# Routing of tokens to experts: a list built on one engine, four token tiles in one counting product, and a new order of steps

## What is computed

```
logits = x @ w_gate                      # 3072 x 8
order = argsort(-logits.flatten())
for idx in order:                        # best pairs first
    tok, e = idx // E, idx % E
    if assigned[tok] >= 0 or counts[e] >= cap:   # cap = 3072 / 8 = 384
        continue
    assigned[tok] = e; counts[e] += 1
for e in range(E):
    h = maximum(x[mask_e] @ w1[e], 0)    # 384 x 1024
    out[mask_e] = h @ w2[e]
```

## Time and profile before

| | |
|---|---|
| median of three runs | 1098.96 us (1096.31 to 1099.07) |
| the profiled execution's own time | 1096.0 us |
| its span, first to last instruction | 1094.1 us |
| attention and MLP end, routing begins | about 713 us |
| first product of expert 0 | 750.48 us |
| last product of expert 7 | 1090.1 us |
| PE busy, share of the span | 96% |

### The profile page before, as it was taken

The page is one execution under the profiler, slowest core; times in us unless marked ns, Lnnn a source line. Parts: engine busy times, 40 slices in busy tenths (PEclk is TensorE's granted clock), DMA queues, the critical chain, the costliest instruction groups (busy, mean ns, idle before and its releaser), DMA issues. The chain is left out here.

```text
span 1094.1 us, 20341 instructions
## 1 busy us (share of the span) xinstructions
PE 1051.4 (96%) x7545; PEld 899.0 (82%) x7545; DVE 596.2 (54%) x2182; ACT 460.4 (42%) x1172; POOL 422.1 (39%) x472
## 2 busy tenths in 40 slices
PE   8899999999999999999999999948999998999998
PEld 7688888888888888888888888837777786878987
DVE  6754747474746465655656554366665765654110
ACT  5765444444444444444444432303333333334442
POOL 1363222222222222222222224206387547486873
PEclk9999999999999999999999999959999999999999
DMA  6663112121212121212111000014244343323520
GB/s 197 209 205 134 56 56 74 53 71 41 70 55 74 55 68 40 71 55 72 51 63 38 29 11 20 1 29 175 90 161 164 125 164 118 128 104 124 203 107 29
DMA packets 24594, 98.20 MB, mean 90 GB/s; under 512 B 4352, under 2 KB 6400, under 8 KB 22304
## 3 DMA queue, kind: packets, MB, share of 16 engines
q0 software_dynamic: 9824, 58.99, 15.3%
q1 hardware_dynamic: 14672, 37.91, 10.6%
HBM read 84.30 MB, written 12.85 MB: 89 GB/s over the span
## 5 line engine op out<-in xcount | busy, mean ns | idle before, releaser
L427 POOL TENSOR_TENSOR g_low<-g,g_high 128x256 fp32r<-128x256 f32 x192 | 155.1, 808 | 470.8 <-ACT g_high L646 470.7
L536 PE MATMUL up_ps<-x_high,w_high 128*128 128x256 f32 x768 | 227.7, 296 | 0.0
L536 PE MATMUL up_ps<-x_low,w_high 128*128 128x256 f32 x768 | 216.1, 281 | 0.0
L536 PE MATMUL up_ps<-x_high,w_low 128*128 128x256 f32 x768 | 215.1, 280 | 0.0
L814 DVE SCALAR_TENSOR_TENSOR g<-g,up_ps 128x256 f32<-128x256 f32 x192 | 80.4, 419 | 237.0 <-ACT g L639 237.0
L646 ACT ACTIVATE g_high<-g 128x256 fp32r<-128x256 f32 x192 | 80.3, 418 | 209.8 <-PE down_ps L549 140.6
L536 PEld LDWEIGHTS up_ps<-x_high,w_high 128*128 128x128 f32 x768 | 144.5, 188 | 10.7 <-issue 7.7
L549 PE MATMUL down_ps<-w_high,g_high 128*128 128x512 f32 x384 | 152.1, 396 | 0.6 <-POOL g_low L427 0.6
L549 PE MATMUL down_ps<-w_high,g_low 128*128 128x512 f32 x384 | 151.4, 394 | 0.0
L549 PE MATMUL down_ps<-w_low,g_high 128*128 128x512 f32 x384 | 151.2, 394 | 0.0
L536 PEld LDWEIGHTS up_ps<-x_low,w_high 128*128 128x128 f32 x768 | 144.8, 188 | 2.7
(11 more groups left out here) (224 smaller groups left out, 1826.8 us busy)
## 6 DMA issues: line engine op xcount, KB each, us to landing
qk_t<-qk_rows SPq DMA_DIRECT2D x20, 720.0 KB, 4.3
v_w<-v_win SPq DMA_DIRECT2D x40, 232.0 KB
w_raw<-weights SPq DMA_DIRECT2D x16, 512.0 KB, 5.5
x_rest<-x_any POOLq DMA_DIRECT2D x24, 256.0 KB, 3.0
x_rows<-x POOLq DMA_DIRECT2D x12, 512.0 KB, 3.2
w_raw<-gate_rows SPq DMA_DIRECT2D x1, 2048.0 KB, 7.2
qk_t<-qk_rows SPq DMA_DIRECT2D x3, 512.0 KB, 4.5
v_w<-v_win SPq DMA_DIRECT2D x8, 128.0 KB
```

The lines of the kernel that those rows point to most:

```text
L427: pool.tensor_tensor(g_low[:, u % 2, :], g[:, u % 2, :], g_high[:, u % 2, :].bitcast(F32), ALU.subtract)\
L536: last = nc.tensor.matmul(up_ps[:, u % 2, 0:GT * P], a[:, f, w], x[:, grp % 2, c, :], start=k == 0, stop=k == 3 * C - 1)
```

## The change

- **Lists.** `keep_list` writes the list to `token_index` by four reductions, one per 32 partitions, in every round. `tokens_kept`, SP's DMAs, PE's spreading product, the masks in `Tables` and `keep_first_tokens` go.
- **Counts.** From round 1 on four tiles make one product (`PACK` = 128 / 32 = 4): 6 products of 128 x 32 in place of 12 of 64 x 16. The result lies in four diagonal blocks, which `find_reached` joins by three subtractions.
- **Digits per expert.** The maximum over experts moves behind the digit's product: `enough` (in bf16) says for each mark and expert whether it is reached, the product gives 8 digits, and `move_key` takes their maximum (`digit`) first. In the last level `margins` keeps the differences, which `count_wins` multiplies in place of `enough`.
- **Places.** `gaps_of` has new distances; there are two slots from count to digit from round 2 on. The lists stand at 0.37, 1.30, 2.23, 3.16, 4.9, 5.2 and 5.15. From SUMS to LIST there are 7 slots, where there were 9 or 11.
- **GpSimd.** w1 is fetched ahead of f = 5, 4, 2 for experts 1 to 3 and of f = 1 after, tokens ahead of f = 8, 6, 5 and 3.
- `keep_busy(17)` stands behind LIST, where it stood behind NEXT.

```diff
@@ -1254,23 +1235,19 @@
...
-        counts_at = route_ps[0:2 * REACH, 0:2 * E]
-        first_counts = route_ps[0:REACH, 0:E]
-        second_counts = route_ps[REACH:2 * REACH, E:2 * E]
-        digit_at = route_ps[:, 16:17]
-        wins_at = route_ps[:, 32:32 + 2 * E]
+        counts_at = route_ps[:, 0:PACK * E]
+        digit_at = route_ps[:, 32:32 + E]
+        wins_at = route_ps[:, 40:40 + 2 * E]
...
-        spread_at = route_ps[:, 256:256 + COLUMNS]
...
-        second_known = sem("second_known")
-        margin_known = sem("margin_known")
+        digit_found = sem("digit_found")
...
@@ -1312,14 +1286,10 @@
...
         def gaps_of(r):
-            ends = [2, 4] + [4, 1, 1] + [3 if r in (1, 3) else 5, 1, 2]
+            ends = [2, 3] + [3, 1, 1] + [2, 1, 2]
             if r == 1:
-                return [4, 2] + [2, 1] * (UPPER - 1) + [3, 1] + [2, 1] * (NL - UPPER - 1) + ends
-            if r == 2:
-                return [5, 1] + [3, 1] * 2 + [2, 1] * (UPPER - 3) + [3, 1] + [2, 1] * (NL - UPPER - 1) + ends
-            if r == 3:
-                return [5, 1] + [3, 1] * (UPPER - 1) + [4, 1] + [2, 1] * (NL - UPPER - 1) + ends
-            return [5, 2] + [3, 1] * (UPPER - 1) + [4, 1] + [3, 1] * (NL - UPPER - 1) + ends
+                return [2, 2] + [3, 1] * (UPPER - 2) + [2, 1, 3, 1] + [2, 1] * (NL - UPPER - 1) + ends
+            return [4, 2] + [3, 2] * (UPPER - 2) + [2, 2, 3, 2] + [2, 2] * (NL - UPPER - 1) + ends
...
@@ -1375,10 +1345,7 @@
...
-                if p == 0:
-                    pool.wait_ge(token_index_ready, 1)
-                else:
-                    pool.wait_ge(tokens_moved, 16 * BLOCKS * p)
+                pool.wait_ge(token_index_ready, p + 1)
...
@@ -1394,9 +1361,9 @@
...
-                if p + 1 < E and f == {0: FC, 1: 4}.get(p, 0):
+                if p + 1 < E and f == {0: FC, 1: 5, 2: 4, 3: 2}.get(p, 1):
                     fetch_w1(p + 1)
-                if p + 1 < E and f == {0: FC, 1: FC, 2: 6}.get(p, 0):
+                if p + 1 < E and f == {0: FC, 1: FC, 2: 6, 3: 5}.get(p, 3):
                     fetch_tokens(p + 1)
...
@@ -1429,17 +1396,6 @@
...
-        @block.sync
-        def _(sp):
-
-            for r in range(1, E):
-                sp.wait_ge(tokens_ready, r + 1)
-                if r > 1:
-                    sp.wait_ge(tokens_moved, 16 * BLOCKS * (r - 1))
-                for k in range(BLOCKS):
-                    sp.dma_start(token_index[k * LIST_ROWS:(k + 1) * LIST_ROWS, r, :],
-                                 tokens_kept[:, r % 2, k * CT:(k + 1) * CT]).then_inc(tokens_moved, 16)
...
@@ -1450,31 +1406,32 @@
...
-                for t in range(0, T, 1 if r == 0 else 2):
+                for t in range(0, T, 1 if r == 0 else PACK):
                     if t in (0, EARLY):
                         pe.wait_ge(compared, (r * NL + lv) * 2 + t // EARLY + 1)
                     if r == 0:
-                        last = nc.tensor.matmul(first_counts[0:reach, :], cmp[:, t, 0:reach], wants[:, t, :], start=t == 0,
+                        last = nc.tensor.matmul(counts_at[0:reach, 0:E], cmp[:, t, 0:reach], wants[:, t, :], start=t == 0,
                                                 stop=t == T - 1)
                     else:
-                        last = nc.tensor.matmul(counts_at, cmp[:, t:t + 2, :].rearrange("p t m -> p (t m)"),
-                                                wants[:, t:t + 2, :].rearrange("p t e -> p (t e)"), start=t == 0,
-                                                stop=t == T - 2)
+                        last = nc.tensor.matmul(counts_at, cmp[:, t:t + PACK, :].rearrange("p t m -> p (t m)"),
+                                                wants[:, t:t + PACK, :].rearrange("p t e -> p (t e)"), start=t == 0,
+                                                stop=t == T - PACK)
                 last.then_inc(counted, 1)
 
-            def digit(r, lv):
+            def find_digit(r, lv):
+
+
                 pe.wait_ge(enough_known, r * NL + lv + 1)
-                nc.tensor.matmul(digit_at, reached_any[:, 0:1].broadcast_to([P, P]), steps_col[:, lv:lv + 1], start=True,
-                                 stop=True).then_inc(digit_known, 1)
+                nc.tensor.matmul(digit_at, steps_col[:, lv:lv + 1].broadcast_to([P, P]), enough[:, :], start=True, stop=True)\
+                    .then_inc(digit_known, 1)
 
             def count_wins(r):
 
 
                 pe.wait_ge(sides_ready, r + 1)
-                reach = LEVELS[NL - 1][0]
                 for k in range(2):
-                    last = nc.tensor.matmul(wins_at[:, k * E:(k + 1) * E], sides[0:reach, k:k + 1].broadcast_to([reach, P]),
-                                            enough[0:reach, :], start=True, stop=True)
+                    last = nc.tensor.matmul(wins_at[:, k * E:(k + 1) * E], sides[:, k:k + 1].broadcast_to([P, P]),
+                                            margins[:, :], start=True, stop=True)
...
@@ -1494,27 +1451,19 @@
...
-            def spread_tokens(r):
-
-
-                pe.wait_ge(tokens_ready, r + 1)
-                nc.tensor.matmul(spread_at, spread[:, :], tokens[:, :], start=True, stop=True).then_inc(tokens_spread, 1)
...
-                elif k == NEXT and r == 0:
-                    spread_tokens(r)
...
@@ -1592,7 +1541,7 @@
...
-                if k == NEXT:
+                if k == LIST:
                     keep_busy(17)
...
@@ -1666,7 +1615,8 @@
...
-            for a in (closed, dead, assigned):
+
+            for a in (closed, dead, assigned, margins, enough):
                 v.memset(a[:, :], 0.0)
             v.memset(places[:, :], float(CAP)).then_inc(places_known, 1)
...
@@ -1706,31 +1656,32 @@
...
                 dve.wait_ge(counted, r * NL + lv + 1)
-                if r == 0:
-                    v.tensor_tensor_reduce(out=enough[0:reach, :], in0=first_counts[0:reach, :], in1=places[0:reach, :],
-                                           scale=1.0, scalar=-BIG, op0=ALU.subtract, op1=ALU.max,
-                                           accum_out=margin[0:reach, :]).then_inc(margin_known, 1)
+
+                missing = places[0:reach, :]
+                for k in range(PACK - 1 if r else 0, 0, -1):
+                    at_k = slice(k * REACH, k * REACH + reach)
+                    to = short[(k - 1) * REACH:(k - 1) * REACH + reach, :]
+                    link(v.tensor_tensor(to, places[at_k, :] if k == PACK - 1 else short[at_k, :],
+                                         counts_at[at_k, k * E:(k + 1) * E], ALU.subtract))
+                    missing = short[0:reach, :]
+                if lv == NL - 1:
+                    link(v.tensor_tensor(margins[0:reach, :], counts_at[0:reach, 0:E], missing, ALU.subtract))
+                    v.tensor_scalar(enough[0:reach, :], margins[0:reach, :], 0.0, None, ALU.is_ge).then_inc(enough_known, 1)
                 else:
-                    v.tensor_tensor(second_enough[0:reach, :], second_counts[0:reach, :], places[REACH:REACH + reach, :],
-                                    ALU.subtract).then_inc(second_known, 1)
-                    dve.wait_ge(second_known, (r - 1) * NL + lv + 1)
-                    v.tensor_tensor_reduce(out=enough[0:reach, :], in0=first_counts[0:reach, :],
-                                           in1=second_enough[0:reach, :], scale=1.0, scalar=-BIG, op0=ALU.add,
-                                           op1=ALU.max, accum_out=margin[0:reach, :]).then_inc(margin_known, 1)
-                dve.wait_ge(margin_known, r * NL + lv + 1)
-                v.tensor_scalar(reached_any[0:reach, :], margin[0:reach, :], 0.0, None, ALU.is_ge)\
-                    .then_inc(enough_known, 1)
+                    v.tensor_tensor(enough[0:reach, :], counts_at[0:reach, 0:E], missing, ALU.is_ge).then_inc(enough_known, 1)
 
             def move_key(r, lv):
 
                 dve.wait_ge(digit_known, r * NL + lv + 1)
+                v.tensor_reduce(digit[:, :], digit_at, AX, ALU.max).then_inc(digit_found, 1)
+                dve.wait_ge(digit_found, r * NL + lv + 1)
                 if lv == NL - 1:
 
-                    v.tensor_scalar(key[:, :], key[:, :], digit_at, 1.0, ALU.subtract, ALU.add).then_inc(key_moved, 1)
-                    v.tensor_scalar(sides[:, 0:1], own, digit_at, -1.0, ALU.subtract, ALU.is_equal)
-                    v.tensor_scalar(sides[:, 1:2], own, digit_at, 0.0, ALU.subtract, ALU.is_equal).then_inc(sides_ready, 1)
+                    v.tensor_scalar(key[:, :], key[:, :], digit[:, :], 1.0, ALU.subtract, ALU.add).then_inc(key_moved, 1)
+                    v.tensor_scalar(sides[:, 0:1], own, digit[:, :], -1.0, ALU.subtract, ALU.is_equal)
+                    v.tensor_scalar(sides[:, 1:2], own, digit[:, :], 0.0, ALU.subtract, ALU.is_equal).then_inc(sides_ready, 1)
                 else:
-                    v.tensor_scalar(key[:, :], key[:, :], digit_at, None, ALU.subtract).then_inc(key_moved, 1)
```

(45 more changed lines are left out.)

21 lines of the change are left out of this document (2 added, 19 removed).

## The result

| | before | after |
|---|---|---|
| median of four runs each, same chip | 1097.74 us (1096.31 to 1099.07) | 1079.79 us (1078.76 to 1080.13) |
| profiled execution's own time, and span | 1096.0, 1094.1 us | 1080.13, 1078.4 us |
| ratio, 95% interval | | 0.9835 (0.9817 to 0.9853) |

A forecast was written before the change was run, and what follows sets the result against it. The prediction took PE's time from 713 us on as the bound. Its terms summed to -10.4 us, from 1096.0 to 1085.6, or 1088.6 as a median; it took 1087, range 1080 to 1095.

The forecast's parts named there:

- Counts: PE's count products, rounds 1 to 6: six wide ones for twelve gain 0.11 us on each of 42 levels, -4.6 us.
- The 0.25 of issue before them stays: PE ahead of a count's loads: the 0.25 us of issue was taken as unchanged by the wider products.
- 64 more add about 0.014: Count load pitch: growth of 0.007 us from 32 to 64 columns extended to 128, giving 0.045, six of them 0.27.
- the bound from below: Count load pitch at least 0.025 us, from the lists' 32-column products: 0.15 for six, gain 0.23 a level, -9.7 us.
- DVE's chain and the distances: DVE between count, digit and key in the experts: longer chain set against new slot distances, -2.1 us in sum.
- The rule of slots: Charged PE waits where a digit or count stands on an up tile's last slot, where DVE runs hidden_low first.
- Lists: PE at the lists: seven slots from mark sums to list bring waits in rounds 2 to 5 and 7, +3.5 us.
- GpSimd: Down products of experts 3 and 5: waits for w_low go through earlier lists and moved fetches, -6.3 us.
- Round 0: Uncovered routing before the first up product: shorter levels and list, -0.9 us, between 0 and -2.
- Wide loads are dear: Rival at the six count products: 0.11 us each, so counts cost +12, total +6.2, 1102 to 1105; chance 0.06.
- More than forecast: Rival: count loads at 0.03 us and no list waits, 1078 to 1081; chance 0.12.
- DVE did become a wait: Rival: PE waits for DVE 0.25 us more on each of 42 levels, +10.5, 1096 to 1099; chance 0.11.

The follow-up runs named there:

- b_wide: Kernel before, its 12 count products a level reading four tiles, so 128 stationary columns in place of 64: 1089.47 us, ratio 0.9955.
- a_pack2: Changed kernel with two tiles a count product again (12 products, 64 columns, one joining subtraction in place of three): 1089.50 us, ratio 0.9957.
- a_oldgaps: Changed kernel with the distances (`gaps_of`) of the kernel before: 1085.76 us, ratio 0.9897.
- b_lists: Kernel before with lists written by four DVE reductions, without SP's DMAs and the spreading product; fetch places as before: 1088.92 us, ratio 0.9940.
- a_head: Changed kernel where ACT rounds four of eight parts of the first w1, then expert 0's tokens, then the other four: 1078.65 us, ratio 0.9832.
- a_twice: Changed kernel with every count in twelve products of 128 columns in place of six: 1083.87 us, ratio 0.9907.
- a_widelist: Changed kernel with the lists' 24 products on 128 stationary columns too, same number of products: 1079.54 us, ratio 0.9848.

## Why the prediction missed

The sign and the places were right; the size was off by 5.3 us of span (-15.7 for -10.4), and the medians (-18.0) show some 2 us more than the profiled pair. The measured 1079.79 us lies just under the stated 1080 to 1095.

- **Counts, forecast -4.6, measured -16.8 before waits.** This is the step that failed, in two halves. A count gained 0.40 us, not 0.11. "The 0.25 of issue before them stays" took the fixed cost of a count as unchanged: with 128 columns the idle ahead of the loads falls only to 0.16, but the product no longer starts late and the next f32 product follows at once, which is 0.17 us a count, as `b_wide` and `a_pack2` show in both directions. And "64 more add about 0.014" was drawn as a line through 32 and 64 columns; at 128 the pitch is 0.024, no more than at 32, which is 0.12 a count. With the bound from below (0.025) and the fixed cost gone, the term is 42 x 0.40. Why the fixed cost goes isn't shown by any run. The lists (32 columns to 128, 0.17 less) and the wins' products (17 rows to 128, 0.27 less) lost it too, so in all three it goes with a stationary that fills the array.
- **DVE's chain and the distances, forecast -2.1, measured +3.1** (counts' waits +4.2, digits -1.1). The rule of slots was applied to counts as long as forecast. A count 0.3 us shorter than forecast leaves DVE that much less time; `b_wide` shows 4.0 us of such waits with DVE's chain as before, and `a_pack2` 7 with the chain changed too. So the surplus of the counts, 12.2, was paid back by 5.2 here. `a_oldgaps` shows that without the new distances it would have been about 6 us more.
- **Lists, forecast +3.5, measured +3.2**, in the rounds named and none in 1 and 6. Right.
- **GpSimd, forecast -6.3, measured -5.1.** Right in that the waits of experts 3 and 5 went, and SP's hop was their cause (`b_lists`). The prediction also counted on the new places of the fetches; they add nothing that a run shows.
- **Round 0, forecast -0.9, measured +0.9.** From DVE's first routing instruction to the first up product it is 37.59 us for 36.65. Of this, 0.30 is round 0 itself: the fetch of w1 comes that much later in it. The levels gained nothing, since the key is as slow as before. The last level was put at nothing and cost 0.21; by the prediction's own links (0.20 less to PE, 0.20 for the subtraction, 0.13 for the reduction) it would have been 0.13. The reductions are 0.17 apart, not 0.1, and the list's end comes 0.2 later, not 0.9 sooner; the list's products ran at a granted clock of 0.50 (739.90 to 740.60) where it was 1.00 before, and in `a_head`, where it was 1.00 again, the list's end is at 27.8 as before. "These steps release GpSimd's fetch, so the saving goes on to the first product" was wrong besides: ACT's rounding of w1 stands in front. The largest part, 0.75, is w1, rounded 9.38 us behind its fetch for 8.63 before (and the product then followed 0.1 sooner). With the same round 0 it is 8.62 in `a_pack2` and 8.59 in `a_twice`, so this part isn't shown to be an effect of the change.
- **Rivals.** "Wide loads are dear" fell: 0.024 a load, far under its 0.085. "More than forecast" (1078 to 1081) has the measured time in it, in part by luck: it named the right term and a load near the measured one, but kept the fixed cost of a count and wanted no list waits, and these two errors offset each other. DVE did become a wait, and still didn't decide.

## What to carry to other kernels

Where short products stand between long ones, price a switch by the step between the long ones' starts, and look for rows whose stationary fills the array before drawing a line through narrower ones: here filling it was worth 0.24 us a switch with twelve products, more than halving their number (0.16), and 0.17 for a list. A gain on the engine that sets the time is paid back in part by what was hidden behind it, so forecast the waits again with the new lengths. And for a first product, list all that it waits for; the last releaser of a fetch isn't the last of the product.

## What the runs showed of the hardware

- bf16 loads in a stream on PE at the full granted clock: pitch 0.025 us with 32 columns (24 moving), 0.031 with 64 (16 moving), 0.024 with 128 (32 moving) and 0.025 with 128 (16 or 24 moving). At a granted clock of 0.50, in round 0, the list's loads stand 0.027 apart with 32 columns and 0.037 with 128 (`after`, `a_widelist`).
- Beyond its pitches such a stream between f32 products with full 128 x 128 stationaries costs PE 0.2 us with 32 or 64 columns and 0.02 with 128. Four f32 products on 17 rows and 128 columns cost 0.27 more than on 128 rows.
- From GpSimd's fetch of w1 (an indirect DMA) to ACT's first rounding of it: 8.5 to 9.7 us over fourteen executions.
- A reduction on 32 partitions of 6 PSUM columns costs DVE 0.17 us each in a row of four. A `tensor_scalar` of 128 x 24 takes 0.25 us with its scalar from SBUF and 0.26 with it from PSUM (718.49, and 718.87 in the earlier trace rows), and the next instruction starts 0.29 behind it both times.
